# Two attention steps at a time in the prologue, and the second MLP's quotient held in PSUM

## The chip, the core and the metric

One core of one Trainium2 chip. The metric is the device time of one execution in microseconds (us). TensorE does matrix products, VectorE (DVE), ScalarE (ACT) and GpSimd (POOL) elementwise work, SyncE (SP) issues the DMAs. TensorE, VectorE and ScalarE reach PSUM, the accumulators' memory (eight banks of 128 x 512 floats here); all compute engines read SBUF.

## The reference

An attention layer followed by two MLPs. Attention: 2 batches, 8 heads, 768 positions, head size 64.

```python
scores = scale * q @ k.T
keep = (pos_k < n_global) | ((rel >= 0) & (rel < n_local))     # 8 and 96
scores = scores - slope[head] * dist                           # where keep, else -1e9
x = softmax(scores) @ v                                        # -> 1536 x 512
h = x @ w_in1                                                  # 512 -> 2048
x = (max(h, 0) + alpha * min(h, 0)) @ w_out1                   # 2048 -> 512
h = x @ w_in2
P = a0 + a1*h + a2*h**2 + a3*h**3
Q = 1 + |b0|*|h| + |b1|*h**2
out = (P / (Q + 1e-6)) @ w_out2
```

## The kernel before

**Tiling.** The 1536 tokens are three blocks of 512. A block has 4 tiles of 128 tokens and 4 pairs of heads, hence 16 attention steps (`STEPS`). A step reads its own tile of keys and the one before, 256 keys (128 in the first tile of the sequence, steps 0 to 3). Each MLP layer works on a block in 16 units m of 128 hidden features: hidden product h(m), gate g(m), split of g into a rounded part `g_hi` and a rest `g_lo`, output product y(m). Every product is made of three products of rounded parts (hi*hi, hi*lo, lo*hi), so h(m) and y(m) have 12 matmuls of 128 x 512 each.

**Stages.** The prologue does the attention of block 0 alone. Then layer 1 runs over three blocks, with the attention of the next block woven in between the matmuls of the first two, then layer 2 over three blocks. In layer 1 h runs two units ahead of y, in layer 2 three (`AHEAD`).

**Prologue.** `prologue_events` gives one order of events that TensorE, ScalarE and VectorE each follow, in program order. In turn s: transpose of the probabilities of step s-3 (`turn_prob`; TensorE L514, copied to SBUF by ScalarE L710), exponentials of s-1 (`exp`, ScalarE L702), scores of s (`score`, TensorE L500 and L502, with VectorE's shift L946), normalising of s-1 (`norm`, VectorE L954, behind the sum L987 and the inverse L991), output of s-3 (`attend`, TensorE L526, ScalarE L715, VectorE L961). Scores stand in four PSUM banks, transposes and outputs in two places each. ScalarE also makes the bias tables (L695), eight parts for steps 0 to 3 before the first exponential, and four pairs of a second table among steps 1 to 4.

**Loads.** SyncE issues all DMAs in its order: q and k of two steps (L377 to L380, once the scores up to two steps before are done), v (L390, L392, once an earlier step has attended), and pieces of 512 KB of the first layer's weights (L405), four of them at once at the start, the others when GpSimd has freed a stage. GpSimd rounds a piece (L1283) and forms the rest (L1247, L1250), one piece after the other. The last six pieces stand ahead of the q and k of block 1, which are issued in a loop.

**Gate of layer 2** for unit m: ScalarE makes h squared (L753), `q_abs` (L756), `denom` (L760), `numer` (L764) and `p_low` (L768) from the PSUM bank of h(m); GpSimd adds and multiplies them in SBUF (L1257, L1259, L1262); VectorE takes the reciprocal of `denom` (L1042), then forms `g_lo` of the unit before (L1054), then the quotient (L1048); ScalarE rounds the quotient to `g_hi` (L774). The banks of h are used by turns of four.

**Output product** (`output`, L606 and L608): y(m) waits for `g_lo` of m, which is the last part of g, then for each of four accumulator banks j does hi*hi, hi*lo, lo*hi. In the last unit TensorE signals after banks 0 and 1 (`y_half_done`) and at the end; ScalarE (L843) and VectorE (L1142) copy two banks each, and SyncE sends them out (L455).

Of the kernel before, what the change touches and what calls it, by code (L numbers as in the profile page):

```python
# [19 lines left out]
F32 = mybir.dt.float32  # L20
# [3 lines left out]
ALU = mybir.AluOpType  # L24
# [5 lines left out]
P = 128  # L30
# [5 lines left out]
BT = TOK // P  # L36
# [27 lines left out]
def build_program(nc, q, k, v, reach, w_in1, w_out1, alpha, w_in2, w_out2, ab, out):  # L64
    ctx = ExitStack()
    with ctx:
# [61 lines left out]
        negmax = sb("negmax", [P, 2, 2], F32)  # L128
        rowsum = sb("rowsum", [P, 2, 2, 2], F32)
# [20 lines left out]

        def in_block0(ab):
            return isinstance(ab, int)
# [114 lines left out]
        def prologue_events():  # L267


            for s in range(STEPS + 3):  # L270
                if s >= 3:
                    yield "turn_prob", s - 3
                if 1 <= s <= STEPS:
                    yield "exp", s - 1
                if s < STEPS:
                    yield "score", s
                if 1 <= s <= STEPS:
                    yield "norm", s - 1
                if s >= 3:
                    yield "attend", s - 3  # L280
# [75 lines left out]
        def _(sp):  # L356
# [10 lines left out]
            def load_qk(ab, i, batch, t):  # L367
                s = STEPS * ab + i
                slot, early = (i // PAIRS) % 2, in_block0(ab) and i < PAIRS
                two, loaded = slice(i % PAIRS, i % PAIRS + 2), (i % PAIRS) // 2  # L370
                tile = slice(t * P, (t + 1) * P) if isinstance(t, int) else bass.ds(t * P, P)
# [10 lines left out]
            def load_v(ab, i, batch, t):  # L382
                s = STEPS * ab + i
                slot, early = (i // PAIRS) % 2, in_block0(ab) and i < PAIRS
                loaded = (i % PAIRS) // 2
                tile = slice(t * P, (t + 1) * P) if isinstance(t, int) else bass.ds(t * P, P)
# [25 lines left out]
            load_piece(order1, 0, 1)  # L412
# [3 lines left out]
            for i in range(2, 4):  # L416
                load_piece(order1, 0, i)
            def due(i):

                return len(stage1) + (i - 2) * WHOLE // STEPS  # L420


            for i in range(PAIRS, STEPS, 2):
                load_qk(0, i, 0, i // PAIRS)
                for piece in range(due(i - 2), due(i)):
                    load_piece(order1, 0, piece)
                if i > PAIRS:
                    load_v(0, i - 2, 0, (i - 2) // PAIRS)
            load_v(0, STEPS - 2, 0, BT - 1)
            for piece in range(due(STEPS - 2), 2 * PIECES):  # L430
                load_piece(order1, 0, piece)
            with sp.Fori(0, BLOCKS - 1) as blk:
                def tile_at(i):

                    (b0, t0), (b1, t1) = (divmod(BT * r + i // PAIRS, TPB) for r in (1, 2))
                    return blk * (b1 - b0) + b0, blk * (t1 - t0) + t0

                load_qk(blk + 1, 0, *tile_at(0))
                for i in range(2, STEPS, 2):
                    load_qk(blk + 1, i, *tile_at(i))  # L440
                    load_v(blk + 1, i - 2, *tile_at(i - 2))
                load_v(blk + 1, STEPS - 2, *tile_at(STEPS - 2))
# [48 lines left out]
        def _(pe):  # L491
# [68 lines left out]
            def hidden(layer, blk, m, half, order, wait_w):  # L560
# [5 lines left out]
                if half == 0:  # L566
# [21 lines left out]
            def output(layer, blk, m, half, order, wait_w, after):  # L588

                c = MC * (blk + BLOCKS * layer) + m  # L590
                if half == 0 and layer == 1:
                    pe.wait_ge(g2_ready, MC * blk + (m + 1))
                elif half == 0:
                    pe.wait_ge(g_ready, c + 1)
                if half == 0:
                    if wait_w:
                        pe.wait_ge(w_ready, 2 * PIECES * layer + consumed_piece(order, m))
                for j in range(2 * half, 2 * half + 2):
                    if m == 0:
# [754 lines left out]
```

## Time and profile before

| | us |
|---|---|
| median of 3 runs (lowest, highest) | 672.76 (672.68, 672.94) |
| profiled execution, its own time | 673.6 |
| span in the profile | 671.9 |
| TensorE busy | 637.6 (95%) |
| VectorE busy | 500.8 (75%) |
| ScalarE, GpSimd busy | 321.0 (48%), 316.6 (47%) |
| mean granted TensorE clock | 0.988 of full |

Busy time of matmuls overlaps, since they are pipelined: a matmul of 128 x 512 is 0.39 us long and the next starts 0.227 us later. Places in the program are read from the timeline, whose times count from the start of the span. The profiled execution took 0.84 us more than the median.

### The profile page before, as it was taken

To read this page: it belongs to the slowest core of one execution; us is meant where nothing else is said; L and a number is where in the kernel's file an instruction comes from. 1 tells how busy PE (TensorE), PEld (TensorE's weight loads), DVE (VectorE), ACT (ScalarE), POOL (GpSimd) and SP (SyncE) were. 2 spreads that over 40 slices of the span, in tenths; PEclk is the share of its full clock that TensorE was granted. 3 is DMA by queue.
4 is the path that set the end of the run, shared out by engine and by line. 5 is a ranking of instruction groups with operands and counts; after the bars stand their busy time and mean duration, and the time that the engine had idled before them with its cause. 6 is when DMAs were issued, how large, how long until landed. Compare 5 with 4: busy or idle time off the path is not lost.

```text
span 671.9 us, 9562 instructions
## 1 busy us (share of the span) xinstructions
PE 637.6 (95%) x3048; PEld 506.4 (75%) x3048; DVE 500.8 (75%) x763; ACT 321.0 (48%) x664; POOL 316.6 (47%) x225
## 2 busy tenths in 40 slices
PE   3986999999999999999999998999999999999986
PEld 2665777777877777778888886888878887778864
DVE  6673766666376666645455569999989999899994
ACT  5671333333143323222111175777777777777772
POOL 5989200000000000001444486888878888788882
PEclk9997999999999999999999998999999999999998
DMA  6774121111000111010323210000010000100001
GB/s 202 200 232 126 32 52 28 28 45 40 0 27 27 46 36 28 9 48 16 102 95 114 98 32 0 1 1 0 1 63 0 0 0 0 62 1 0 1 0 65
DMA packets 38931, 31.26 MB, mean 47 GB/s; under 512 B 9008, under 2 KB 33264, under 8 KB 38896
## 3 DMA queue, kind: packets, MB, share of 16 engines
q1 hardware_dynamic: 38896, 30.83, 15.2%
q8 instruction: 18, 0.29, 0.2%
q14 instruction: 17, 0.14, 0.1%
HBM read 27.67 MB, written 3.15 MB: 46 GB/s over the span
## 4 chain that ended last, share of the span: by engine, by line
PE 76%; POOL 9%; ACT 5%; issue 3%; DMA 3%; SPq 2%; DVE 1%; POOLq 0%; ACTq 0%; DVEq 0%
PE ps_h L583 26%; PE ps_y L606 19%; PE ps_y L608 13%; PE ps_s L535 4%; POOL denom L1257 4%; POOL numer L1259 4%; PE ps_s L583 3%; PE ps_o L556 3%; PE ps_o L583 2%; DMA kT<-in_k 2%; PE ps_o L545 2%; ACT denom L760 2%; PE ps_y L502 2%; ACT h_sq L753 1%; SPq L377 1%
## 5 line engine op out<-in xcount | busy, mean ns | idle before, releaser
L1042 DVE RECIPROCAL denom<-denom 128x512 f32<-128x512 f32 x48 | 160.4, 3341 | 10.2 <-POOL denom L1257 10.2
L1250 POOL TENSOR_TENSOR win_lo<-stage,win_hi 128x1024 fp32r<-128x1024 f32 x8 | 19.2, 2402 | 265.4 <-DVE win_hi L1019 265.4
L583 PE MATMUL ps_h<-xy_hi,win_hi 128*128 (+1 forms) x288 | 119.2, 414 | 0.7 <-DVE xy_lo L961 0.7
L583 PE MATMUL ps_h<-xy_lo,win_hi 128*128 (+1 forms) x288 | 113.1, 393 | 0.0
L583 PE MATMUL ps_h<-xy_hi,win_lo 128*128 (+1 forms) x288 | 112.9, 392 | 0.0
L1257 POOL TENSOR_TENSOR denom<-denom,q_abs 128x512 f32<-128x512 f32 x48 | 79.0, 1646 | 39.5 <-ACT denom L760 39.5
L740 ACT ACTIVATE g_hi<-g 128x512 fp32r<-128x512 f32 x48 | 30.3, 631 | 138.3 <-PE ps_y L606 128.6
L608 PE MATMUL ps_y<-wout_hi,g_hi 128*128 128x512 f32 x192 | 77.7, 405 | 8.8 <-DVE g_lo L1054 8.8
L1036 DVE TENSOR_TENSOR g_lo<-g,g_hi 128x512 fp32r<-128x512 f32 x48 | 33.5, 697 | 65.9 <-ACT g_hi L740 65.9
L1259 POOL TENSOR_TENSOR numer<-numer,h_sq 128x512 f32<-128x512 f32 x48 | 80.3, 1672 | 3.7 <-ACT numer L764 3.7
L606 PE MATMUL ps_y<-g_hi,wout_hi 128*128 128x512 f32 x192 | 80.8, 421 | 0.0
L1048 DVE TENSOR_TENSOR numer<-numer,denom 128x512 f32<-128x512 f32 x48 | 76.5, 1593 | 0.1
L608 PE MATMUL ps_y<-wout_hi,g_lo 128*128 128x512 f32 x192 | 76.4, 398 | 0.0
L608 PE MATMUL ps_y<-wout_lo,g_hi 128*128 128x512 f32 x192 | 76.1, 397 | 0.0
L606 PE MATMUL ps_y<-g_lo,wout_hi 128*128 128x512 f32 x192 | 75.2, 392 | 0.0
L606 PE MATMUL ps_y<-g_hi,wout_lo 128*128 128x512 f32 x192 | 75.1, 391 | 0.0
L1262 POOL TENSOR_TENSOR numer<-numer,p_low 128x512 f32<-128x512 f32 x48 | 63.5, 1323 | 3.8
L583 PEld LDWEIGHTS ps_h<-xy_hi,win_hi 128*128 128x128 f32 x288 | 54.6, 190 | 14.1 <-issue 2.7
L583 PEld LDWEIGHTS ps_h<-xy_hi,win_lo 128*128 128x128 f32 x288 | 54.4, 189 | 11.7
L583 PEld LDWEIGHTS ps_h<-xy_lo,win_hi 128*128 128x128 f32 x288 | 54.5, 189 | 10.2
L1027 DVE TENSOR_SCALAR g<-ps_h,alpha_sb 128x512 f32<-128x512 f32 x48 | 36.0, 750 | 28.9 <-PE ps_h L583 28.9
L608 PEld LDWEIGHTS ps_y<-wout_hi,g_hi 128*128 128x128 f32 x192 | 36.6, 191 | 23.0 <-DVE g_lo L1054 16.1
(138 smaller groups left out, 1170.5 us busy)
## 6 DMA issues: line engine op xcount, KB each, us to landing
stage<-in_w_in SPq DMA_DIRECT2D x8, 512.0 KB, 3.4
stage<-in_w_out SPq DMA_DIRECT2D x8, 512.0 KB, 3.3
qT<-in_q SPq DMA_DIRECT2D x48, 64.0 KB, 2.4
kT<-in_k SPq DMA_DIRECT2D x24, 128.0 KB, 2.3
vv<-in_v SPq DMA_DIRECT2D x24, 128.0 KB, 2.2
out<-xy_raw SPq DMA_DIRECT2D x12, 256.0 KB, 2.2
xy_raw<-in_w_in SPq DMA_DIRECT2D x4, 512.0 KB, 5.7
xy_raw<-in_w_out SPq DMA_DIRECT2D x4, 512.0 KB, 5.6
```

Source lines behind the costliest of these rows:

```text
L535: mm = pe.matmul(ps_s[:, 2 * P * h:2 * P * (h + 1)], qT[:, pair, h, :], kT[:, pair].rearrange("d s t -> d (s t)"), start=True, stop=True)
L583: mm = pe.matmul(ps_h_at(layer, m), w[:, kc, cut], x[:, blk, kc, :], start=(kc == 0 and n == 0), stop=(kc == KC - 1 and n == 2))
L606: mm = pe.matmul(ps_y[:, j, :], w[:, m, cut], g[:, m % 2, :], **flags)
L608: mm = pe.matmul(ps_y[:, j, :], g[:, m % 2, cut], w[:, m, :], **flags)
L740: act.activation(g_hi[:, m % 2, :], g1[:, :], ACT.Copy).then_inc(g_hi_ready, 1)
L1027: dve.tensor_scalar(g1[:, :], ph, 0.0, alpha_sb[:, m:m + 1], ALU.min, ALU.mult).then_inc(neg_part, 1)
L1036: dve.tensor_tensor(g_lo[:, m % 2, :], g1[:, :], g_hi[:, m % 2, :].bitcast(F32), ALU.subtract).then_inc(g_ready, 1)
L1042: dve.reciprocal(denom[:, r, :], denom[:, r, :]).then_inc(inverse_ready, 1)
L1048: dve.tensor_tensor(numer[:, r, :], numer[:, r, :], denom[:, r, :], ALU.mult).then_inc(ratio_ready, 1)
L1257: pool.tensor_tensor(under, under, q_abs[:, :], ALU.add).then_inc(denom_ready, 1)
L1259: pool.tensor_tensor(top, top, h_sq[:, :], ALU.mult).then_inc(numer_high, 1)
L1262: pool.tensor_tensor(top, top, p_low[:, :], ALU.add).then_inc(numer_ready, 1)
```

## The change

Four things are edited.

1. The prologue's events come for two steps at a time: both transposes, both exponentials, both scores, both norms, both outputs. A step is transposed and attended in the turn of two after its norm. `negmax` and `rowsum` get four places instead of two. ScalarE makes four parts of the first bias table before the first exponential, the other four among the exponentials of steps 0 and 1, and the second table among those of steps 2 to 5. VectorE's preparation of the second distance table is cut in two (`later_keep`, `later_distances`).
2. SyncE's program has no loop: all three blocks of loads are written out, one weight piece at the start, then one piece per two steps in block 0 and two per two steps in block 1, behind the q, k and v of the turn.
3. An output product does its eight matmuls with `g_hi` first and waits only for `g_hi`; the four with `g_lo` come last, behind a wait for `g_lo`. `y_half_done` is signalled after the lo matmul of bank 1.
4. In layer 2 the reciprocal, the quotient and the source of `g_hi` and `g_lo` are in the PSUM bank of h(m), no longer in `denom` and `numer`. The reciprocal therefore waits for ScalarE's last read of that bank (`h_read`); ScalarE may write `denom` after the reciprocal and `numer` after the quotient of two units before; h(m+4) waits for `g_lo` of m.

```diff
-            for s in range(STEPS + 3):
-                if s >= 3:
-                    yield "turn_prob", s - 3
-                if 1 <= s <= STEPS:
-                    yield "exp", s - 1
...
+            for s in range(0, STEPS + 4, 2):
+                for i in (0, 1):
+                    if s >= 4:
+                        yield "turn_prob", s - 4 + i
+                for i in (0, 1):
+                    if 2 <= s <= STEPS:
+                        yield "exp", s - 2 + i
+                for i in (0, 1):
+                    if s < STEPS:
+                        yield "score", s + i
+                for i in (0, 1):
+                    if 2 <= s <= STEPS:
+                        yield "norm", s - 2 + i
+                for i in (0, 1):
+                    if s >= 4:
+                        yield "attend", s - 4 + i
...
+            piece = 1
+            for at_block in range(BLOCKS):
+                for i in range(0 if at_block else PAIRS, STEPS + 2, 2):
+                    if i < STEPS:
+                        load_qk(at_block, i, *divmod(BT * at_block + i // PAIRS, TPB))
+                    if i > (0 if at_block else PAIRS):
+                        load_v(at_block, i - 2, *divmod(BT * at_block + (i - 2) // PAIRS, TPB))
+                    if i < STEPS:
+                        for _ in range(2 if at_block else 1):
+                            if piece < 2 * PIECES:
+                                load_piece(order1, 0, piece)
+                                piece += 1
...
-                        pe.wait_ge(h_read, c2 - 3)
+                        pe.wait_ge(g2_ready, c2 - 3)
...
+                passes = [(j, w, g_hi) for j in range(KC) for w in (wout_hi, wout_lo)] + [(j, wout_hi, g_lo) for j in range(KC)]
+                for n in range(half * len(passes) // 2, (half + 1) * len(passes) // 2):
+                    j, w, g = passes[n]
+                    if m == 0 and n in (0, 2, 4, 6):
...
+                    if n == 2 * KC and layer == 1:
+                        pe.wait_ge(g2_ready, MC * blk + (m + 1))
...
+                    if after is None and m == MC - 1 and n == 2 * KC + 1:
+                        mm.then_inc(y_half_done, 1)
...
-                    act.wait_ge(ratio_ready, u - 1)
+                    act.wait_ge(inverse_ready, u - 1)
...
-                    act.wait_ge(g2_ready, u - 1)
+                    act.wait_ge(ratio_ready, u - 1)
...
-            for head in range(HEADS):
+            for head in range(4):
                 first_bias(head, slice(3 * P, 4 * P), D_FIRST)
...
-                if what == "exp" and 1 <= arg <= PAIRS:
+                if what == "exp" and arg < 2:
+                    for head in (2 * arg + 4, 2 * arg + 5):
+                        first_bias(head, slice(3 * P, 4 * P), D_FIRST)
+                elif what == "exp" and arg < 2 + PAIRS:
...
-                dve.reciprocal(denom[:, r, :], denom[:, r, :]).then_inc(inverse_ready, 1)
+                dve.wait_ge(h_read, MC * blk + (m + 1))
+                dve.reciprocal(ps_h_at(1, m), denom[:, r, :]).then_inc(inverse_ready, 1)
...
-                dve.tensor_tensor(numer[:, r, :], numer[:, r, :], denom[:, r, :], ALU.mult).then_inc(ratio_ready, 1)
+                dve.tensor_tensor(ps_h_at(1, m), numer[:, r, :], ps_h_at(1, m), ALU.mult).then_inc(ratio_ready, 1)
```

**TensorE in the full-width part of the prologue.** Before, one step after another (here the transposes of step 5, the scores of step 8, the outputs of step 5; then 6, 9, 6):

```order
L514 MATMUL ps_s<-ident,prob 128x128 [waits probT_ready,prob_ready]
L514 MATMUL ps_s<-ident,prob 128x128 x3
L502 MATMUL ps_y<-kT,qT 128x256 [waits prob_ready,qk_in0]
L502 MATMUL ps_y<-kT,qT 128x256
L526 MATMUL ps_o<-xy_raw,vv 64x128 [waits x_ready,v_in0,probT_ready]
L526 MATMUL ps_o<-xy_raw,vv 64x128 x3
L514 MATMUL ps_h<-ident,xy_raw 128x128 [waits probT_ready,prob_ready]
L514 MATMUL ps_h<-ident,xy_raw 128x128 x3
L502 MATMUL ps_y<-kT,qT 128x256 [waits prob_ready,qk_in0]
L502 MATMUL ps_y<-kT,qT 128x256
L526 MATMUL ps_h<-probT,vv 64x128 [waits x_ready,v_in1,probT_ready]
L526 MATMUL ps_h<-probT,vv 64x128 x3
```

Now (transposes of steps 4 and 5, scores of 8 and 9, outputs of 4 and 5):

```order
L500 MATMUL ps_h<-ident,prob 128x128 [waits probT_ready,prob_ready]
L500 MATMUL ps_h<-ident,prob 128x128 x3
L500 MATMUL ps_s<-ident,prob 128x128 [waits probT_ready,prob_ready]
L500 MATMUL ps_s<-ident,prob 128x128 x3
L488 MATMUL ps_y<-kT,qT 128x256 [waits prob_ready,qk_in0]
L488 MATMUL ps_y<-kT,qT 128x256
L488 MATMUL ps_y<-kT,qT 128x256 [waits prob_ready,qk_in0]
L488 MATMUL ps_y<-kT,qT 128x256
L512 MATMUL ps_h<-probT,vv 64x128 [waits x_ready,v_in0,probT_ready]
L512 MATMUL ps_h<-probT,vv 64x128 x3
L512 MATMUL ps_o<-xy_raw,vv 64x128 [waits x_ready,v_in0,probT_ready]
L512 MATMUL ps_o<-xy_raw,vv 64x128 x3
```

The groups of two steps stand together, and the transposes of a step come one turn of two after its norm.

**SyncE at the end of the prologue's loads.** Before, from the last v of block 0 to the first q of block 1, which is in the loop:

```order
L390 DMA vv<-in_v 128x256 [waits attended]
L392 DMA vv<-in_v 32x256
L405 DMA xy_raw_lo<-in_w_in 128x4x256 [waits w_ready]
L405 DMA xy_raw_lo<-in_w_out 128x2x512 [waits w_ready]
L405 DMA xy_raw<-in_w_in 128x4x256 [waits w_ready]
L405 DMA xy_raw<-in_w_out 128x2x512 [waits w_ready]
L405 DMA xy_raw_lo<-in_w_in 128x4x256 [waits w_ready]
L405 DMA xy_raw_lo<-in_w_out 128x2x512 [waits w_ready]
L432 UNCONDITIONAL_BRANCH
L432 ISA
L377 ISA [waits scored]
```

Now:

```order
L392 DMA vv<-in_v 128x256 [waits attended]
L394 DMA vv<-in_v 32x256
L379 DMA qT<-in_q 64x2x128 [waits scored]
L379 DMA qT<-in_q 64x2x128
L380 DMA kT<-in_k 128x2x128
L382 DMA kT<-in_k 128x2x32
L407 DMA xy_raw_lo<-in_w_out 128x2x512 [waits w_ready]
L407 DMA xy_raw<-in_w_in 128x4x256 [waits w_ready]
L379 DMA qT<-in_q 64x2x128 [waits scored]
```

Six pieces, each behind a wait for GpSimd, stood ahead of block 1's first q and k; now none of the last nine does.

**An output product of layer 2 on TensorE.** Before:

```order
L608 MATMUL ps_y<-wout_hi,g_hi 128x512 [waits g2_ready]
L608 MATMUL ps_y<-wout_hi,g_lo 128x512
L608 MATMUL ps_y<-wout_lo,g_hi 128x512
L608 MATMUL ps_y<-wout_hi,g_hi 128x512
L608 MATMUL ps_y<-wout_hi,g_lo 128x512
L608 MATMUL ps_y<-wout_lo,g_hi 128x512
```

The other six rows repeat these. Now:

```order
L599 MATMUL ps_y<-wout_hi,g_hi 128x512 [waits g2_hi_ready]
L599 MATMUL ps_y<-wout_lo,g_hi 128x512
L599 MATMUL ps_y<-wout_hi,g_hi 128x512
L599 MATMUL ps_y<-wout_lo,g_hi 128x512
L599 MATMUL ps_y<-wout_hi,g_hi 128x512
L599 MATMUL ps_y<-wout_lo,g_hi 128x512
L599 MATMUL ps_y<-wout_hi,g_hi 128x512
L599 MATMUL ps_y<-wout_lo,g_hi 128x512
L599 MATMUL ps_y<-wout_hi,g_lo 128x512 [waits g2_ready]
L599 MATMUL ps_y<-wout_hi,g_lo 128x512 x3
L569 MATMUL ps_h<-xy_hi,win_hi 128x512 [waits g2_ready]
```

The wait at the front is for `g_hi`; the one for `g_lo` stands behind eight of the twelve matmuls.

## Rows read from the trace of the kernel before

**Rows 1.** Timeline, prologue: start us, length us, engine, line, operation, count [idle before].

```profile
25.38 0.66 PE L514 MATMUL ps_h<-ident,prob 128*128 128x128 f32 x4
...
33.57 0.66 PE L514 MATMUL ps_h<-ident,prob 128*128 128x128 f32 x4
...
34.06 1.03 PE L502 MATMUL ps_y<-kT,qT 128*128 128x256 f32 x4
...
34.22 0.16 DVE L991 RECIPROCAL rden<-den 128x2 f32<-128x2 f32 x1
34.26 0.60 ACT L710 ACTIVATE probT<-ps_h 128x512 f32<-128x512 f32 x1 [0.29 <-PE ps_h L514]
34.48 0.69 DVE L954 TENSOR_TENSOR prob<-ps_y,rden 128x512 f32<-128x512 f32 x1
...
35.02 0.67 PE L526 MATMUL ps_h<-probT,vv 128*64 128x128 f32 x8
...
35.57 0.21 ACT L702 ACTIVATION_READ_ACCUMULATOR ps_y<-ps_y,negmax 128x1 f32 x1
...
46.76 0.66 PE L514 MATMUL ps_h<-ident,xy_raw 128*128 128x128 f32 x4
```

**Rows 2.** Timeline: first 256-key scores, and the second bias table on ScalarE.

```profile
17.74 2.08 PE L502 MATMUL ps_y<-kT,qT 128*128 128x256 f32 x4 [4.08 <-DMA kT<-in_k]
...
22.28 0.94 ACT L695 ACTIVATE bias<-dist 128x384 bf16<-128x384 bf16 x2
```

**Rows 3.** Timeline: end of the prologue and first attention step of the loop.

```profile
52.05 0.50 PE L583 MATMUL ps_h<-xy_hi,win_hi 128*128 128x512 f32 x1 [0.71 <-DVE xy_lo L961]
...
60.95 2.07 PE L535 MATMUL ps_s<-kT,qT 128*128 128x256 f32 x4 [4.49 <-DMA kT<-in_k]
...
62.46 0.99 PE L583 MATMUL ps_h<-xy_hi,win_hi 128*128 x1
```

**Rows 4.** Timeline of layer 2, third block: one unit on VectorE.

```profile
645.41 3.34 DVE L1042 RECIPROCAL denom<-denom 128x512 f32<-128x512 f32 x1
...
648.67 0.62 DVE L1054 TENSOR_TENSOR g_lo<-numer,g_hi 128x512 fp32r<-128x512 f32 x1
...
649.22 1.77 DVE L1048 TENSOR_TENSOR numer<-numer,denom 128x512 f32<-128x512 f32 x1
```

**Rows 5.** Timeline of the turn from layer 1 to layer 2.

```profile
396.36 1.73 DVE L1054 TENSOR_TENSOR g_lo<-numer,g_hi 128x512 fp32r<-128x512 f32 x1 [1.21 <-ACT g_hi L774]
...
397.62 1.62 POOL L1262 TENSOR_TENSOR numer<-numer,p_low 128x512 f32<-128x512 f32 x1
...
398.01 2.47 DVE L1066 TENSOR_TENSOR xy_lo<-ps_y,xy_hi 128x512 fp32r<-128x512 f32 x4
...
404.69 0.63 ACT L774 ACTIVATE g_hi<-numer 128x512 fp32r<-128x512 f32 x1 [3.38 <-DVE numer L1048]
...
407.84 1.20 DVE L1054 TENSOR_TENSOR g_lo<-numer,g_hi 128x512 fp32r<-128x512 f32 x1
...
410.28 2.19 DVE L1130 TENSOR_TENSOR wout_lo<-stage,wout_hi 128x1024 fp32r<-128x1024 f32 x1
```

**Rows 6.** Waits of TensorE, 63 us to the end: total us, times, longest us.

```profile
PE ps_y L608 <- DVE g_lo L1054: 8.8, 5, 3.1
```

**Rows 7.** Critical chain around the same turn: start us, us, what.

```profile
409.09 4.62 PE ps_y L608 x12
...
419.34 2.72 PE ps_s L583 x12
```

**Rows 8.** Timeline of TensorE, start of the second block of layer 2.

```profile
499.44 0.50 PE L608 MATMUL ps_y<-wout_hi,g_hi 128*128 128x512 f32 x1 [1.20 <-DVE g_lo L1054]
```

**Rows 9.** Timeline of the tail.

```profile
654.85 0.50 PE L608 MATMUL ps_y<-wout_hi,g_hi 128*128 128x512 f32 x1 [2.50 <-DVE g_lo L1054]
```

**Rows 10.** Timeline of the tail, VectorE evictions, then the output DMA issues.

```profile
666.13 0.69 DVE L1142 COPY xy_raw<-ps_y 128x512 f32<-128x512 f32 x1 [0.67 <-PE ps_y L608]
```

**Rows 11.** Timeline of the output DMA issues on the SyncE queue.

```profile
665.39 2.20 SPq L455 DMA_DIRECT2D out<-xy_raw  x4
```

More of the change, by code:

```diff
@@ L590, in output @@
                 c = MC * (blk + BLOCKS * layer) + m
[L591 to L594, printed above, removed]
                 if half == 0:
+                    if layer == 1:
+                        pe.wait_ge(g2_hi_ready, MC * blk + (m + 1))
+                    else:
+                        pe.wait_ge(g_hi_ready, c + 1)
                     if wait_w:
                         pe.wait_ge(w_ready, 2 * PIECES * layer + consumed_piece(order, m))
-                for j in range(2 * half, 2 * half + 2):
-                    if m == 0:
+                passes = [(j, w, g_hi) for j in range(KC) for w in (wout_hi, wout_lo)] + [(j, wout_hi, g_lo) for j in range(KC)]
@@ L601, in output @@
+                for n in range(half * len(passes) // 2, (half + 1) * len(passes) // 2):
+                    j, w, g = passes[n]
+                    if m == 0 and n in (0, 2, 4, 6):
                         pe.wait_ge(y_read, (blk + BLOCKS * layer) * KC + (j + 1))
[L602 to L608 removed]
+                    if n == 2 * KC and layer == 1:
+                        pe.wait_ge(g2_ready, MC * blk + (m + 1))
+                    elif n == 2 * KC:
+                        pe.wait_ge(g_ready, c + 1)
+                    flags = dict(start=(m == 0 and n < 2 * KC and n % 2 == 0), stop=(m == MC - 1 and n >= 2 * KC))
+                    cut = slice(j * P, (j + 1) * P)
+                    if layer == 0:
+                        mm = pe.matmul(ps_y[:, j, :], w[:, m, cut], g[:, m % 2, :], **flags)
+                    else:
+                        mm = pe.matmul(ps_y[:, j, :], g[:, m % 2, cut], w[:, m, :], **flags)
+                    if after is None and m == MC - 1 and n == 2 * KC + 1:
+                        mm.then_inc(y_half_done, 1)
@@ L609, in output @@
                 if half == 1:
                     mm.then_inc(y_done, 1)
-                elif after is None and m == MC - 1:
-                    mm.then_inc(y_half_done, 1)
             def run_block(layer, blk, attention, after, wait_w, wait_next):
@@ L1073, in _ @@
                     first_shift(arg, 0)
-                    if arg:
-                        denominator(0, arg - 1)
                     first_shift(arg, 1)
-                    if arg:
-                        inverse(0, arg - 1)
-                    else:
+                    if arg == 1:
+                        later_keep()
+                    if arg == 3:
                         later_distances()
-                elif what == "norm":
-                    if arg == STEPS - 1:
-                        denominator(0, arg)
-                        inverse(0, arg)
+                elif what == "norm" and arg % 2 == 0:
+                    denominator(0, arg)
+                    denominator(0, arg + 1)
+                    inverse(0, arg)
+                    inverse(0, arg + 1)
                     first_normalised(arg)
+                    first_normalised(arg + 1)
                 elif what == "attend":
```

70 lines of the change are left out of this document (17 added, 53 removed).

## Prediction

> **What bounds the kernel now.** I read the page first: TensorE is busy 95% of the span, so only what makes it wait, or run at its low clock, is worth anything. Then its waits, then the chain that ended last, then the timelines of the four places where these put the lost time. The reader is to see there:
>
> - In the prologue TensorE waits 4.08 us for k of step 4 [rows 2], which stands behind four weight pieces in the DMA queue, and at its end 4.49 us for k of block 1 [rows 3], which stands behind six pieces, each with a wait for GpSimd. Between them a step costs (46.76 - 25.38) / 10 = 2.14 us from the transposes of step 4 to those of step 14 [rows 1], close to TensorE's own work in a step: transposes 0.49 (33.57 to 34.06), scores 0.96 (to 35.02), outputs 0.67, together 2.12.
> - From 63 us on TensorE's waits are 8.8 us, five of them, all of y(m) for `g_lo` in layer 2 [rows 6]: 3.1 at the turn from layer 1, 1.20 at the second block [rows 8], 2.50 in the tail [rows 9], the other two 2.0 together.
> - A unit of layer 2 in the second and third block takes VectorE 645.41 to 648.67 for the reciprocal (3.26), 0.55 for `g_lo`, and, the quotient being 1.77 long, about 1.69 until the next one: 5.50 [rows 4]. TensorE needs 2 x 2.72 = 5.44 for h and y [rows 7]. So VectorE sets the pace there, by 0.06 us a unit.
>
> **The change part by part.** All sums are against the profiled execution, 673.6 us with a span of 671.9.
>
> *Quotient in PSUM.* It removes a second SBUF input from the quotient and from `g_lo`. The quotient is 1.77 long while GpSimd computes [rows 4]. The nearest rows with one PSUM and one SBUF input are the four `xy_lo`: 2.47 us together, 0.62 each, although a GpSimd operation ran through their first 1.2 us [rows 5]. I take 0.65 for both new forms; bounds are 0.62 and 1.77. A unit on VectorE becomes 3.26 + 0.65 + 0.65 = 4.56, well under 5.44. A reciprocal that writes PSUM is not in this trace; between no difference and 0.2 us more (that would still leave VectorE 0.7 us under TensorE) I take none. The added wait for `h_read` asks for ScalarE's last read of the bank, 2 x 0.77 or so behind `denom`, while GpSimd still needs 1.3 to 1.7 for its addition to `denom`: hidden. Behind the reciprocal on VectorE stand `g_lo` and the quotient, for which ScalarE and TensorE wait; the cover that pays if I am wrong is the three units that h runs ahead. The wait of h(m+4) for `g_lo` of m costs nothing, since y(m) has just been issued on it.
>
> The Trainium skill, "VectorE: DVE Perf Modes", section on the TRN2 errata, speaks against the move: a VectorE instruction pays a fixed 120 cycles from PSUM and 58 from SBUF. By it quotient and `g_lo` would be longer by 62 cycles of 0.96 GHz, an estimate of 0.06 us each, and a unit 4.7: no change in the sum.
>
> *Output product hi first.* y(m) can begin with `g_hi` and needs `g_lo` only 8 matmuls, 1.81 us, later.
>
> At the turn: `g_hi` of unit 1 is there at 404.69 + 0.63 = 405.32 [rows 5], y(1) began at 409.09 and took 4.62 us instead of 2.72, at the low clock [rows 7]. It can now follow h(4) at about 405.9. The first `g_lo`, 1.73 long [rows 5], falls to 0.65, which pulls all that VectorE does behind it 1.0 us forward, so `g_lo` of unit 1 ends near 409.0 - 1.0 - 0.6 = 407.4, in time. y(1) ends at 408.6, h(5) at 411.3. Late next is `g_lo` of unit 2: behind 407.4 VectorE has a quotient 0.65, a rounding of weights 0.7, `wout_lo` 2.19 [rows 5], a reciprocal 3.26 and itself 0.65: 414.9. y(2) ends 0.9 later, at 415.8, where it ended at 419.34 before [rows 7]. Gain 3.5.
>
> From there TensorE has 42 h and 45 y, 87 x 2.72 = 236.6 us. Before, from 419.34 to the last matmul's end, when VectorE's last eviction began at 666.13 [rows 10], less about 0.1, it took 246.7. The difference of 10.1 is the two waits at block starts and the slack 0.06 x 28 units, the two waits of the tail, and low clock after the 2.50 wait. All have their cover now but the last: behind the end of h(15), y(12) to y(14) take 8.16, and the chain of unit 15 is 3.35 to GpSimd's sum, 3.26, 0.65, 0.65 and 0.75 for `g_hi`: 8.65. So 0.5 stays, gain 9.6. Sum for layer 2: -13.1.
>
> *Tail.* `y_half_done` moves from 6 matmuls before the end to 2, that is 0.9 us later; the four output DMAs take SyncE 2.20 [rows 11], which started 0.7 before the end of y and will start 0.2 behind it. Cost +0.9.
>
> *Loads.* k of step 4 now follows one piece, not four: its scores start near 13.3 instead of 17.74 (-4.4). Block 1's k no longer waits: the 4.49 us go, and the low clock after them, scores 1.51 instead of 0.96 (60.95 to 62.46 [rows 3]) and some 1.3 us in the h behind: 6.3 us in all. Pieces come later, but none before it is needed: piece 8 is due at unit 6, 40 us into the loop, and I expect GpSimd done with it by 62 us.
>
> *Pairs.* Here the change costs. In a full-width turn of two, ScalarE does two copies and two steps of exponentials between the transposes of one turn and the norm of the same turn, and the next turn's transposes wait for that norm. From rows 1: transposes to the first copy 34.26 - 33.57 = 0.69; copy and exponentials of one step 34.26 to 35.78 = 1.52, twice 3.04; two sums and two inverses, 0.16 each and 0.26 from the second inverse to the norm, 0.55; the norm 0.69; together 5.0. TensorE's work in a turn is 4.1 to 4.2 and does not set the end. Before, norm and transposes lay a whole turn further apart, so this chain was covered. Five such turns from step 4 to step 14: 25.1 against 21.4, +3.7. The two turns before it carry the second bias table, 4 x 0.94 [rows 2], on the same ScalarE chain: 5.0 + 1.9 + shifts 0.2 = 7.1 for the second; from 13.3 I get the transposes of step 2 at 18.8 (at half speed, as the 2.08 of [rows 2] against 1.03) and those of step 4 at 25.9, against 25.38. So the DMA gain at the start is used up (+0.5 net), and 52.05 [rows 3] becomes 56.3. The 18 matmuls behind it take 4.4, then block 1's scores follow at once: 60.7, where before the loop began at 60.95 and lost 1.85 to the clock, as if at 62.8. Net for prologue and loads: -2.1. The unknown is the turn of two: bounds 4.1 (TensorE alone) and 5.9 (k of the turn after next is issued only after outputs, v and a piece: 3.7 of issue, then 2.4 to 4.0 to land), hence 56 or 65 for the loop's start.
>
> Sum: 673.6 - 13.1 + 0.9 - 2.1 = 659.3. The median of the runs lies 0.84 under the profiled execution, so 658.5.
>
> **Rivals.**
> - *Pairs as fast as TensorE.* If ScalarE's exponentials overlap its copies more than rows 1 show, a turn is 4.1 to 4.2: 5 x 0.9 less, 654.0. Against it: in rows 1 ScalarE works back to back from 34.26 to 35.78.
> - *Loads set the turn.* 5.9 a turn gives 5 x 0.9 more, 663.0. For it: 4.08 and 4.49 us of waits for k already [rows 2, 3]. Against: fewer pieces at once.
> - *The port is not freed.* If GpSimd still stretches the quotient to 1.77, VectorE stays at 5.5 a unit; the 1.7 of slack, and about 2 in the tail, come back: 662.2. Against it the `xy_lo` of [rows 5].
> - *The other side: the prologue stays at the low clock.* Each turn leaves TensorE idle for 0.9 of 5.0 us. Should the clock therefore not rise, a step is 0.98 + 1.92 + 1.2 = 4.1 and a turn 8.2; over six turns +19, giving 677.7. It decides from 2.4 us a turn on. Against it: at half speed the same work would fill the turn, and full-width scores went from 2.08 to 1.03 [rows 1, 2] once the work was dense.
>
> The Trainium skill, "TensorE: Matmul & The Clock Gate", section on the HAM clock gate, says the clock is set by how busy the array has been recently and halves after idleness. Trace and rule agree at the turn, where a wait of 3.1 us was followed by 4.62 for 12 matmuls [rows 6, 7]; for idle pieces of 0.9 us no run here shows it, and this rival is what the rule makes of them if they count.
>
> **How the numbers follow.** Forecast as summed 0.55 (its own range 656 to 661.5), fast pairs 0.14, loads 0.17, port 0.08, low clock 0.04, and 0.02 for a loss of another kind. Range 653.5 to 664: it takes in the first three rivals. This kernel's measurement tells 0.2% from no change, 1.3 us. Faster 0.95, within 0.01, slower 0.04.
>
> **What would show it.** Right: in layer 2 the quotient 0.65 to 0.7 long everywhere, y and h at 2.72 each in all three blocks, a TensorE wait of 1 to 2 us inside y(2) for `g_lo` and less than 1 in the tail; in the prologue turns of 5 us with TensorE idle before the transposes, waiting for the norm; no wait at the loop's start. Wrong: transposes every 4.1 us per two steps, or waits for k; a quotient still at 1.7; matmuls at 1.2 GHz in the middle of the prologue; waits for `w_ready` in the loop, because GpSimd starts later.

## The result

| | median us (lowest, highest) | ratio to the kernel before, 95% interval |
|---|---|---|
| kernel before | 672.83 (672.68, 672.94) | |
| changed kernel | 666.18 (665.79, 666.53) | 0.9901 [0.9884, 0.9918] |

Faster by 6.65 us; forecast were 14.3 and a range of 653.5 to 664.0. The direction was right, the size was not, and the time lies outside the range. The profiled execution took 666.53 us with a span of 664.8, beside 673.6 and 671.9 before: -7.1 in either.

### The profile page after: what moved, and what is told of

Its sections match the earlier page's. It is cut to its first block, busy times and chain, and to the rows that moved or that the text cites. A ratio compares the mean times of both kernels' runs of the same rounds, so it can differ in the third digit from the quotient of the medians.

```text
span 664.8 us, 9458 instructions
## 1 busy us (share of the span) xinstructions
PE 633.5 (95%) x3048; PEld 509.8 (77%) x3048; DVE 466.2 (70%) x763; ACT 311.6 (47%) x664; POOL 283.1 (43%) x225
## 4 chain that ended last, share of the span: by engine, by line
PE 85%; DVE 6%; ACT 3%; issue 3%; POOL 2%; DMA 0%; DVEq 0%; POOLq 0%; ACTq 0%
PE ps_h L569 28%; PE ps_y L597 19%; PE ps_y L599 18%; PE ps_s L569 5%; PE ps_o L569 5%; PE ps_s L521 4%; PE ps_o L542 3%; PE ps_o L531 2%; ACT ps_y L693 1%; PE ps_y L488 1%; PE ps_h L500 1%; POOL numer L1258 1%; PE ps_s L500 1%; ACT bias L686 1%; DVE ps_y L944 1%
## 5 line engine op out<-in xcount | busy, mean ns | idle before, releaser
L1041 DVE RECIPROCAL ps_h<-denom 128x512 f32<-128x512 f32 x24 | 80.6, 3360 | 17.4 <-POOL denom L1256 16.9
L1256 POOL TENSOR_TENSOR denom<-denom,q_abs 128x512 f32<-128x512 f32 x48 | 63.0, 1312 | 69.7 <-ACT denom L751 69.7
L599 PE MATMUL ps_y<-wout_hi,g_hi 128*128 128x512 f32 x192 | 74.8, 390 | 0.0
L599 PE MATMUL ps_y<-wout_lo,g_hi 128*128 128x512 f32 x192 | 74.7, 389 | 0.0
L1258 POOL TENSOR_TENSOR numer<-numer,h_sq 128x512 f32<-128x512 f32 x48 | 62.0, 1292 | 0.0
L599 PE MATMUL ps_y<-wout_hi,g_lo 128*128 128x512 f32 x192 | 51.7, 391 | 2.1 <-DVE g_lo L1053 2.1
L719 ACT ACTIVATE probT<-ps_o 128x512 f32<-128x512 f32 x32 | 19.0, 594 | 73.7 <-PE ps_o L531 73.7
L1041 DVE RECIPROCAL ps_s<-denom 128x512 f32<-128x512 f32 x12 | 40.3, 3360 | 16.9 <-POOL denom L1256 16.7
L597 PE MATMUL ps_y<-g_lo,wout_hi 128*128 128x512 f32 x192 | 51.8, 392 | 0.0
```

The source lines that it names most:

```text
L597: mm = pe.matmul(ps_y[:, j, :], w[:, m, cut], g[:, m % 2, :], **flags)
L599: mm = pe.matmul(ps_y[:, j, :], g[:, m % 2, cut], w[:, m, :], **flags)
L1041: dve.reciprocal(ps_h_at(1, m), denom[:, r, :]).then_inc(inverse_ready, 1)
L1256: pool.tensor_tensor(under, under, q_abs[:, :], ALU.add).then_inc(denom_ready, 1)
L1258: pool.tensor_tensor(top, top, h_sq[:, :], ALU.mult).then_inc(numer_high, 1)
```

## The profile after

TensorE's row of the page and the clock granted to it, in 40 slices of 16.6 us each:

```profile
PE   3788999999999999999999999899999999999996
...
PEclk8798999999999999999999999899999999999998
```

The second and the fourth slice of the clock are at 7 and 8, inside the prologue. TensorE's waits over the whole span (total us, times, longest us):

```profile
PE ps_h L500 <- DVE prob L952: 10.6, 4, 5.5
PE ps_y L486 <- DMA kT<-in_k: 5.4, 1, 5.4
PE ps_h L500 <- DVE xy_raw L952: 4.5, 4, 2.2
PE ps_y L599 <- DVE g_lo L1053: 2.1, 2, 1.9
PE ps_o L531 <- DVE prob L994: 1.6, 3, 0.7
PE ps_h L569 <- DVE xy_lo L959: 0.7, 1, 0.7
```

Of k only the first load is waited for; the waits of [rows 2, 3] are gone. The 8.8 us of [rows 6] are 2.1. In their place stand 15.1 us of transposes waiting for the norm, in eight turns. The prologue on TensorE, timeline (transposes and scores; some rows of each turn left out):

```profile
14.71 0.66 PE L500 MATMUL ps_h<-ident,prob 128*128 128x128 f32 x2 [5.51 <-DVE prob L952]
...
15.59 3.62 PE L488 MATMUL ps_y<-kT,qT 128*128 128x256 f32 x8
...
20.93 0.44 PE L500 MATMUL ps_h<-ident,xy_raw 128*128 128x128 f32 x2 [0.88 <-DVE xy_raw L952]
...
27.27 1.12 PE L500 MATMUL ps_h<-ident,prob 128*128 128x128 f32 x4 [3.26 <-DVE prob L952]
...
29.03 3.62 PE L488 MATMUL ps_y<-kT,qT 128*128 128x256 f32 x8
...
34.62 0.66 PE L500 MATMUL ps_h<-ident,xy_raw 128*128 128x128 f32 x4 [0.54 <-DVE xy_raw L952]
...
39.57 0.66 PE L500 MATMUL ps_h<-ident,prob 128*128 128x128 f32 x4 [0.89 <-DVE prob L952]
...
49.47 0.66 PE L500 MATMUL ps_h<-ident,prob 128*128 128x128 f32 x4 [0.89 <-DVE prob L952]
...
54.28 1.11 PE L500 MATMUL ps_h<-ident,xy_raw 128*128 128x128 f32 x4 [2.20 <-DVE xy_raw L952]
```

From step 6 to step 12 a turn is (49.47 - 34.62) / 3 = 4.95 us with 0.89 idle: the forecast of 5.0. Three places are not as forecast: the scores of step 4, at 15.59 and not 13.3, behind transposes that waited until 14.71; the turn from step 4 to 6, 7.35 us with scores at half speed; and the transposes of step 14, again slow. Behind them h(0)'s second half, at 52.05 before [rows 3], starts at 60.20 and not at 56.3. The clock granted from step 4's transposes on (columns: stretch, its length, busy us and count of TensorE, its weight loads, VectorE, ScalarE, GpSimd, then the mean granted clock as a share of 2.4 GHz, DMA share, GB/s):

```profile
27.20:34.60 7.40, 6.81 (x32) 5.38 (x32) 3.76 (x18) 3.57 (x12) 4.47 (x3) 0.58 0.26 79
34.60:54.20 19.60, 14.68 (x120) 11.14 (x120) 13.21 (x57) 13.83 (x48) 10.18 (x6) 0.99 0.58 171
54.20:57.20 3.00, 2.92 (x16) 2.30 (x16) 1.02 (x4) 1.19 (x2) 1.31 (x2) 0.50 1.07 343
```

Behind the 3.26 and the 2.20 us of idle TensorE is at or near its lower level of 1.2 GHz; between them, with 0.89 idle in each turn, at 2.4. What was late at 14.71, timeline of VectorE and GpSimd:

```profile
10.26 2.39 DVE L917 TENSOR_SCALAR xy_raw_lo<-xy_raw_lo,nn 128x32 f32<-128x32 f32 x1
10.27 2.34 POOL L1249 TENSOR_TENSOR win_lo<-xy_raw,win_hi 128x1024 fp32r<-128x1024 f32 x1
```

An operation on 32 columns, 0.24 us long before, ends with GpSimd's tensor_tensor that began beside it. The same operation and GpSimd's first piece in the kernel before, timeline:

```profile
8.32 0.24 DVE L919 TENSOR_SCALAR xy_raw_lo<-xy_raw_lo,nn 128x32 f32<-128x32 f32 x1
...
9.57 1.04 POOL L1283 CAST win_hi<-xy_raw 128x1024 fp32r<-128x1024 f32 x1 [6.76 <-DMA xy_raw<-in_w_in]
10.69 2.35 POOL L1250 TENSOR_TENSOR win_lo<-xy_raw,win_hi 128x1024 fp32r<-128x1024 f32 x1
```

GpSimd's two operations moved forward by 0.42 us, VectorE's moved back by 1.94: it now stands behind the shift of step 3 (`later_distances`), and stood behind that of step 0.

In layer 2 a unit of the third block on VectorE reads as follows (before: [rows 4]):

```profile
633.86 3.36 DVE L1041 RECIPROCAL ps_h<-denom 128x512 f32<-128x512 f32 x1 [0.90 <-POOL denom L1256]
637.13 0.67 DVE L1053 TENSOR_TENSOR g_lo<-ps_o,g_hi 128x512 fp32r<-128x512 f32 x1
637.72 0.68 DVE L1047 TENSOR_TENSOR ps_h<-numer,ps_h 128x512 f32<-128x512 f32 x1
```

The quotient fell from 1.77 to 0.68, and VectorE idles 0.90 us in each 5.44. The turn from layer 1, the chain that ended last (before: [rows 7]; at the end of layer 1 the kernel before is 3.0 us earlier, its h at 389.70 and not 392.69):

```profile
414.17 3.35 DVE ps_o L1041
417.52 0.59 DVE g_lo L1053
418.11 0.04 issue
418.16 1.34 PE ps_y L599 x4
419.49 4.19 PE ps_s L569 x12
423.69 2.73 PE ps_y L599 x12
```

y(2) ends at 419.5; the h behind it takes 4.19 instead of 2.72 us. The tail (before: [rows 10, 11]):

```profile
658.03 1.29 DVE L1141 COPY xy_raw<-ps_y 128x512 f32<-128x512 f32 x2 [1.88 <-PE ps_y L599]
658.65 2.05 SPq L441 DMA_DIRECT2D out<-xy_raw  x4
```

Both banks of VectorE are copied in one go, and SyncE starts behind TensorE's end: from the start of VectorE's last copy to the span's end it is 6.8 us, where it was 5.8. Part of that can be scatter between traces: with the old order it is 6.3 in e1, with the new one 7.2, 7.4 and 7.0 in e2, e3 and e9.

The 7.1 us of span are therefore: end of layer 1 3.0 later (a forecast of 2.1 earlier), layer 2 11.1 shorter (13.1), tail 1.0 longer (0.9).

## The experiments

Twelve kernels were measured in three groups, e1 to e4, e5 to e8 and e9 to e12, each beside the kernel before. That kernel had medians of 674.1 to 674.5 us there, over 1 us above its first ones, so kernels of different groups are compared by their ratio to it, and steps by their traces. "Single" stands for attention steps one at a time in the prologue, as before.

| | us | ratio, 95% interval |
|---|---|---|
| e1 before + PSUM quotient | 669.54 | 0.9927 [0.9901, 0.9953] |
| e2 before + g_hi first | 671.60 | 0.9955 [0.9939, 0.9971] |
| e3 both | 664.16 | 0.9842 [0.9810, 0.9874] |
| e4 both, new loads (all but the pairs) | 653.35 | 0.9676 [0.9647, 0.9704] |
| e5 changed kernel, GpSimd waits | 664.15 | 0.9841 [0.9819, 0.9862] |
| e6 e5 + bias table early | 660.76 | 0.9785 [0.9757, 0.9812] |
| e7 e4, GpSimd waits | 652.61 | 0.9669 [0.9649, 0.9688] |
| e8 e4, last weights later | 649.93 | 0.9632 [0.9613, 0.9651] |
| e9 e7 and e8 together | 649.55 | 0.9630 [0.9611, 0.9649] |
| e10 e9, pieces later | 650.94 | 0.9651 [0.9632, 0.9671] |
| e11 e9, banks 0 and 1 earlier | 650.15 | 0.9637 [0.9616, 0.9658] |
| e12 changed kernel again | 665.72 | 0.9874 [0.9849, 0.9898] |

**e1, e2, e3: the parts of layer 2.** e1 takes the hunks of the diff on `inverse2`, `ratio2`, `split2` and their waits, e2 the one on `output`, e3 both.

> The kernel before with only the quotient, reciprocal and source of g_hi and g_lo moved to PSUM; prologue, loads and output order as before. Theory A (VectorE's pace is what layer 2 loses, and the second SBUF input is what slows the quotient): the quotient falls from 1.77 to 0.65-0.70 us everywhere, the waits of y for g_lo shrink from 8.8 to about 4 (the turn from layer 1 stays), 672.8 - 8.5 = about 664.3 us. Rival B (the order of y is what matters, since it moves the moment at which g_lo is wanted): the quotient is shorter but y still waits, 670 or more.

> The kernel before with only the order of the output product changed (g_hi matmuls first, g_lo last, y_half_done before the last two matmuls). Theory A: VectorE still needs 5.5 us a unit against 5.44 of TensorE, so the 1.8 us of later demand are gained once, at the end, less 0.9 for the later y_half_done, and some low clock after long waits goes: about 670.5 to 671.5 us. Rival B: the order carries the gain, 666 or less.

> The kernel before with both edits of the MLP part (PSUM quotient, g_hi first), its prologue and its loads unchanged. Theory A (the shortfall of the prediction lies mostly in the prologue): layer 2 and tail give what the profile after shows there, -11.1 + 1.0 = -10.1: 662.7 us, that is faster than the changed kernel at 666.2, so the new prologue with its loads is a loss of 3.5. Rival B (the prologue part is worth the 2.1 that was forecast and layer 2 gives less than its traces show, for instance because the turn is different when it comes at another time): 668 us.

e1 gave half of what was expected, 4.6 us. The quotient is 0.68 long everywhere, but y still waits 7.9 us, at the same places as in [rows 6, 8]. TensorE at the second block of e1:

```profile
498.65 0.50 PE L608 MATMUL ps_y<-wout_hi,g_hi 128*128 128x512 f32 x1 [1.26 <-DVE g_lo L1055]
```

That is the 1.20 of [rows 8] with VectorE idle for 0.9 us a unit: the wait at a block's start is not VectorE's pace, but the chain behind one unit, and only a later demand covers it. In e2 the quotient is still 1.77 long, the waits at the block starts are 0.2 and 0.3, and those of the turn and the tail stay. Each alone leaves most waits, together they leave 2.1 us; 4.6 and 2.5 add up to 7.1, together it is 10.0 (against 674.13 in its group). In e3's trace the gain is 9.5 us of span. So layer 2 and the tail give what the trace after says, and prologue and loads together are a loss. The ratios, 0.984 for e3 and 0.990 and 0.987 for the changed kernel (e12), say so with intervals that touch; the traces say it clearly: the last h of layer 1 starts at 389.71 in e3, as in the kernel before, and at 392.69 and 392.28 in the two of the changed kernel.

**e4: without the pairs.** The hunks on `prologue_events`, `negmax`, `rowsum`, the bias parts and the distance tables are left out.

> As the run before, with the new order of loads too, so that only the pairs (two attention steps at a time) are missing from the changed kernel. Theory A: scores of step 4 start near 13.4 us, step 4 to 14 keep 2.14 us a step, block 1's k is there in time: the loop's first scores near 52 us where before lost until an effective 62.8; 662.7 - 10.7 = 652.0 us. Rival B (loads set the turn without pairs): q and k of two steps, 3.7 us of issue and 2.4 to 4.0 to land, come every 5.9 us and not every 4.3, TensorE waits for k again and again: 661 us. Rival C (the pairs cost nothing, and the shortfall lies elsewhere): 666 us.

Theory A: 653.35, expected 652.0. The new loads alone are worth 10.8 us (664.16 to 653.35; forecast 4.4 + 6.3 = 10.7). The pairs cost 0.9901 - 0.9676 = 0.0225, 15 us, by the ratios (13 us with the 0.9874 of e12), and 10.7 between the profiled spans, 664.8 and 654.1, of which e4's is that of its slowest execution. B is seen in small: two waits for k, 1.7 us together. The trace has the collision too, on larger operations:

```profile
8.91 1.30 DVE L907 TENSOR_TENSOR dist<-xy_raw_lo 128x256 bf16<-128x256 f32 x1
10.01 2.39 POOL L1237 TENSOR_TENSOR win_lo<-xy_raw,win_hi 128x1024 fp32r<-128x1024 f32 x1
10.13 2.42 DVE L908 TENSOR_TENSOR dist<-xy_raw_lo 128x128 bf16<-128x128 f32 x1
```

Before, these took 0.42 and 0.28 and were over at 9.54, when GpSimd's first piece began at 9.57. SyncE issues that piece at 5.3 in every trace, but it does not land at one time: with the old load order GpSimd begins it at 9.57, 9.66, 9.75 and 9.85 (before, e1, e3, e2), with the new one, where the landing sets GpSimd's start, at 8.89, 8.91, 9.15, 9.40 and 9.90 (e4, e12, changed kernel, e8, e7).

**e5, e7: the collision taken away.** One line, ahead of GpSimd's pieces, in the changed kernel (e5) and in e4 (e7):

```diff
+            pool.wait_ge(dist_ready, 3)
             for n in range(2 * PIECES):
```

> The changed kernel with one line more: GpSimd does not begin its weight pieces before VectorE has made both distance tables. Theory A (VectorE's small operation on the distances took 2.39 us instead of 0.24 only because a GpSimd tensor_tensor ran beside it): it takes 0.24 again, the first transposes start at 14.71 - 2.15 = 12.6 us, the scores of steps 4 and 5 behind them, everything up to the loop by 2 us earlier, 666.2 - 2.1 = 664 us or the same ratio to the kernel before less 0.003. Rival B (k of step 4, not the norm, would be late next, or the low clock takes it back): 666 us.

> The kernel with everything of the change but the pairs (653.35 us, span 654.1), with GpSimd's wait for the distance tables. Theory A: the two distance operations that took 1.30 and 2.42 us take 0.42 and 0.28, the first transposes start near 10.9 and not 13.91 us; k of step 4 is late next (issued at 7.7, with 2.4 to 4 us to land), so 2.0 to 3.0 us less: 651 us. Rival B (VectorE was not held, or k takes all of it back): no change.

VectorE and TensorE in e5:

```profile
10.45 0.23 DVE L917 TENSOR_SCALAR xy_raw_lo<-xy_raw_lo,nn 128x32 f32<-128x32 f32 x1
...
24.86 1.11 PE L500 MATMUL ps_h<-ident,prob 128*128 128x128 f32 x4 [3.26 <-DVE prob L952]
...
51.87 0.66 PE L500 MATMUL ps_h<-ident,xy_raw 128*128 128x128 f32 x4 [2.20 <-DVE xy_raw L952]
```

0.23 again; the transposes of steps 4 and 14 come 2.4 us earlier than in the changed kernel, the last h of layer 1 2.9 earlier (389.82), and the ratio is 0.006 under that of the changed kernel, 0.003 under e12's, with overlapping intervals there. Theory A. In e7 the first transposes start at 10.88, not 13.91, and the loop's first scores at 50.60, not 54.71, but the median gained 0.7 us only, where 2 to 3 were expected: e8 and e4 have the same prologue, and e8's profiled execution has its first transposes at 10.87. And in e7's own trace the new line held nothing: GpSimd waited for the piece itself, when VectorE's tables had been made 0.4 us before (9.52).

```profile
9.90 1.04 POOL L1271 CAST win_hi<-xy_raw 128x1024 fp32r<-128x1024 f32 x1 [7.10 <-DMA xy_raw<-in_w_in]
```

So without pairs the collision falls out one way or the other, with the landing of the piece, and e7's trace shows an execution that would have escaped it anyway; the line shows at work in e5. With pairs it was there in both profiled executions, which is what e12 was run for:

> The changed kernel itself once more, as a reference on the same chip. Theory A: VectorE's small operation on the distances takes 2.4 us again because GpSimd's first piece is ready at the same moment; ratio to the kernel before 0.989 to 0.991, first transposes at 14.7 us. Rival B (the collision falls out one way or the other from execution to execution, as it did between two of the kernels without pairs): it takes 0.24 here, transposes near 12.6, and the time is 2 us lower.

```profile
10.24 2.16 DVE L917 TENSOR_SCALAR xy_raw_lo<-xy_raw_lo,nn 128x32 f32<-128x32 f32 x1
```

The turn from step 4 to 6 took 6.26 us in this trace and 7.35 in the first, TensorE being back at full clock sooner. 0.9874 against 0.9901 is also how far this ratio moves between two groups; the intervals overlap.

**e6: the idle time before step 4's transposes.** Both distance tables are made behind step 1's shift, and four of the eight parts of the second bias table come where ScalarE idled:

```diff
-                elif what == "exp" and arg < 2 + PAIRS:
+                if what == "exp" and 1 <= arg < 4:
...
-                    for head in (2 * arg - 4, 2 * arg - 3):
+                    for head in (range(4), (4, 5), (6, 7))[arg - 1]:
```

> As the run before, and the second bias table is made earlier: VectorE makes both distance tables in one go behind step 1's shift, ScalarE four pairs of parts behind the exponentials of step 1, where it idled for 5.6 us, and two each behind those of steps 2 and 3. Theory A (the 3.26 us of idle TensorE before the transposes of step 4 came from the bias parts on ScalarE's chain, and the low clock behind it from that idle time): the idle time falls to 0.9 to 1.5 us, the following turn takes 5.0 us and not 7.35, so 1.9 + 2.4 us less than the run before, 660 us. Rival B (the low clock at 27 to 35 us comes from the pairs as such, since each turn idles): the turn stays over 7 us and only 1.9 us are gained.

```profile
22.71 0.66 PE L500 MATMUL ps_h<-ident,prob 128*128 128x128 f32 x4 [1.38 <-DVE prob L952]
...
27.95 0.66 PE L500 MATMUL ps_h<-ident,xy_raw 128*128 128x128 f32 x4 [0.89 <-DVE xy_raw L952]
...
47.61 0.91 PE L500 MATMUL ps_h<-ident,xy_raw 128*128 128x128 f32 x4 [2.20 <-DVE xy_raw L952]
```

Idle 1.38 instead of 3.26, and the turn behind it takes 5.24 instead of 7.34 us (e5: 24.86 to 32.20). Theory A: 2.15 us at step 4's transposes and 2.1 in the turn behind, 4.26 at step 14. The loop gains 3.1 of them (61.04 to 57.97), since behind the 2.20 us of idle the transposes are slow here and were not in e5. With the collision gone, and the low clock too but for the transposes of step 14, the pairs still cost 8.0 us of span against e7 (659.0 and 651.0; ratios 0.9785 and 0.9669).

**e8: the turn to layer 2.** In e4, the last weight piece is rounded and its rest formed in the first block's loop, which is written out, and no longer ahead of it:

```diff
-                elif what == "done":
-
-                    weights(MC - 1)
...
+                        if blk == 0 and arg == 5:
+                            weights(MC - 1)
+                        elif blk == 0 and arg == 8:
```

> The kernel with everything of the change but the pairs, and VectorE rounds the last weight piece of layer 2 behind the gates of units 5 and 8 of the first block, not ahead of unit 3 at the turn. Theory A (the rounding and the rest of that piece, 3.5 us with their gaps, are what makes g_lo of unit 2 late by 1.9 us, and the 1.5 us of low clock behind it come from that wait): the wait and the slow 12 matmuls of 4.19 us go, 3.4 us less, 650 us. Rival B (GpSimd's chain of units 2 and 3 is as late as VectorE's, so g_lo of unit 2 or 3 waits for GpSimd instead): 1 us or less. Rival C (the low clock has another cause than the wait): 2.2 us less, the 4.19 stays.

The chain that ended last in e8, across the turn:

```profile
404.18 2.72 PE ps_s L564 x12
406.90 2.72 PE ps_y L594 x12
409.62 2.72 PE ps_o L564 x12
```

Theory A: no wait, no slow product, and against e7 the last matmuls start 3.1 us earlier (640.55, 643.67).

**e9: both fixes.** e7's line and e8's edit.

> Everything of the change but the pairs, with GpSimd's wait for the distance tables and the last weight piece of layer 2 rounded later. Theory A (the two gains stand in different stages and add): 649.9 less what the collision of the distances costs in the executions that have it, 0.7 in the medians so far (653.35 against 652.61) and 3.1 between the two profiled executions: 649 us, with a narrower spread. Rival B (the collision was not in most executions anyway): 649.9.

649.55, the fastest kernel here, 3.7% under the kernel before; not to be told from e8, whose profiled execution escaped the collision; that most of the others did too is likely (648.8 to 650.6 us, where e4 has 651.2 to 656.0) and not shown.

**e10: fewer issues ahead of k.**

```diff
-                        for _ in range(2 if at_block else 1):
+                        for _ in range(2 if at_block else int(i not in (8, 10))):
```

> As the run before, and no weight piece is issued behind the loads of steps 8 and 10, so SyncE has two issues of 0.47 us less ahead of the k of steps 10 and 12. Theory A (SyncE's issue of nine DMAs a turn, 3.95 of 4.28 us, is what makes k of steps 8 to 11 late by 0.9 to 1.3 us): the wait for k shrinks to under 0.4, 0.9 us less. Rival B (two more pieces then fall into the loop, where GpSimd's work stretches VectorE's operations ahead of the transposes): the waits for prob in the loop grow by as much, no change or 1 us more.

Rival B, by a different row than it named. The waits for k, 0.9 together, are 0.35, and the loop's first scores come 0.87 earlier (51.37 to 50.50); then, VectorE and TensorE:

```profile
50.29 2.53 DVE L1022 TENSOR_TENSOR g_lo<-g,g_hi 128x512 fp32r<-128x512 f32 x1 [0.77 <-ACT g_hi L726]
...
57.45 1.13 PE L516 MATMUL ps_s<-kT,qT 128*128 128x256 f32 x4 [1.81 <-DVE prob L962]
```

`g_lo` takes 2.53 and not 0.69 us, held by a piece of GpSimd (49.90 to 52.27), the next one 1.64, and the scores of step 1 wait 1.81 us for VectorE. The edit did more than move pieces: GpSimd forms the rest of the first eight pieces in one operation of 1024 columns each, and of the later ones in parts of 256. In e9 the piece at this place is a later one, in four parts (50.06 to 53.34), and the same `g_lo`, at 51.16, takes 0.88.

**e11: the tail.**

```diff
+                last = after is None and m == MC - 1
+                if last:
+                    passes = passes[:6] + passes[8:10] + passes[6:8] + passes[10:]
```

> As the first run of this call, but the last output product finishes banks 0 and 1 four matmuls before its end and not two (banks 0 to 2 with g_hi, g_lo of banks 0 and 1, bank 3, g_lo of banks 2 and 3), so that half of the result can leave earlier. Theory A (the 0.9 to 1.0 us of the tail come from y_half_done): the time from TensorE's end to the span's end falls from 6.8 to 6.2-6.4, while the wait for g_lo grows by 0.45, so 0 to 0.3 us less in all. Rival B (the span's end is set by the last two DMAs' landing alone): the wait grows and nothing is gained, 0.4 us more.

SyncE starts its output 0.34 us earlier (641.61, e9 641.95), VectorE's last copy starts 0.57 later (641.89, e9 641.32), spans are 648.4 and 648.3, the ratios overlap: no change. From that copy to the end it is 6.5 us for 7.0, so the order of the last product does set a part of the tail, but this way of getting it back costs as much.

## Why the prediction was wrong

By its own steps, against the profiled executions. It missed by 7.2 us (666.5, forecast 659.3). The step that failed is the net for prologue and loads, put at -2.1 and measured at +3.0. Two terms of it were at nothing: the stretching of VectorE's small distance operation by GpSimd (0.24 us, measured 2.39), and the low clock in the turn from step 4 to 6 (put at 5.0 us, measured 7.35).

1. *Quotient in PSUM*: right. 0.68 and 0.67 us for 0.65 (`g_lo` was 0.62 from SBUF [rows 4], so the 0.06 that the prediction set beside its sum is about there), VectorE needs 5.44 - 0.90 = 4.54 us a unit for 4.56. The rival of the port not freed is out.
2. *The turn from layer 1*: y(2) ended 2.9 us earlier for 3.5 (419.49 against 419.34 + 3.0), with a wait of 1.9 us inside it as foreseen. What was not priced is what this wait does to the clock, though the prediction names the same pair in the kernel before (3.1 us of wait, then 4.62 for a product): the h behind took 4.19 us, +1.5. e8 removed wait and slow product together.
3. *Steady state, boundaries and tail's stall*: gain 9.7 for 9.6, if the 1.5 is left with point 2 (658.03 - 419.49 = 238.5 to VectorE's last copy; before 666.13 - 419.34 = 246.8). But the reason given for the two waits at block starts was wrong in part: e1 shows that VectorE's pace is not their cause, g_hi first is what removes them.
4. *`y_half_done`*: +1.0 for +0.9, as near as traces of one order agree among themselves (5.8 and 6.3, 6.8 to 7.4).
5. *Loads*: right in size, 10.8 for 10.7, where nothing else takes the gain (e4). Loads never set the turn; that rival is out.
6. *Pairs, the turn of two*: 4.95 for 5.0, idle 0.89 for 0.9. The arithmetic of that chain held. Up to the loop's first scores the pairs cost 7.4 us in e6 against e7 (57.97, 50.60), where the forecast implied 60.7 - (62.8 - 10.7) = 8.6; but that one has 1.9 us of bias parts in it, which e6 moved away, and e6 has slow transposes at step 14, so the two agree only roughly.
7. *What it missed in the prologue*, 3.9 us (60.20 for 56.3). (a) +2.1: the distance operation now stands beside GpSimd's first piece, and e5 shows what that costs. Two edits brought them together: the pairs moved the operation back, from 8.32 to 10.26, and the load order can bring the piece forward, here from 9.57 to 9.15. The prediction speaks of neither. The first would have been enough, as far as the rows tell: e5's distance operations run from 10.45 to 11.67, and GpSimd's tensor_tensor at its old place, 10.69 to 13.04, would have met them. No run has the pairs with the old loads. (b) +2.4: the low clock behind the idle time before step 4's transposes. It follows from the prediction's own chain: the turn that ends with these transposes was put at 7.1 us with the bias parts in it, and TensorE's work in a turn is at most 4.2, hence 3 us idle. The rival of the low clock was asked of the turns of 0.9 us idle, where it never came, and priced for six of them alike, not for this one. e6 shows it. (c) +1.0: the same behind step 14's transposes, 5.92 us from there to 60.20 where e5 without it takes 4.91. Stretches shorter than forecast gave 1.6 back, the turn from step 2 to 4 above all, 6.34 for 7.1.
8. *Layer 1 behind it*, 1.2 us more: pieces that GpSimd works on in the loop stretch VectorE there. The transposes wait 1.6 us (0.7 in e3, whose loop has the old loads), behind rows as this one, 0.62 long where GpSimd is idle (at 89.32):

```profile
83.77 1.68 DVE L994 TENSOR_SCALAR prob<-prob,rden 128x256 f32<-128x256 f32 x2
```

"Pieces come later, but none before it is needed" was true and not the point. e10 shows the mechanism, not this size; about 0.3 us of the 1.2 stay unexplained.

Together: 3.9 + 1.2, 1.5 + 0.6 of point 2, and 0.1 of the tail less 0.1 of point 3, 7.2. The range failed because its upper end was the loads' rival, and no case held the collision or the low clock for one turn alone.

The Trainium skill, "SBUF — State Buffer", section "SBUF: two separate sides", says that GpSimd's operations and VectorE's with two SBUF inputs or in a two-port mode exclude each other for a whole instruction, the one that starts first holding the pair. The rows at 10.26 and 10.13 agree, 2.39 and 2.42 us against GpSimd's 2.34 and 2.39, though at 10.26 the two starts are 0.01 us apart and do not tell which was first; by this rule the collision could have been forecast from the new places of the two. For the clock, "TensorE: Matmul & The Clock Gate", section "What's actually happening", says that the same kernel can come out differently from run to run. The two traces of the changed kernel agree: behind the same 3.26 us of idle the turn from step 4 to 6 took 7.35 us in one, with a granted clock of 0.58, and 6.26 in the other (e12), with 0.76.

Not settled: whether the old loads with the pairs would have hidden the pairs' cost or kept the collision (not run), and how often the collision falls in executions that were not profiled.

## What to carry to other kernels

Price an idle piece of TensorE by what runs behind it too: here 3.26 us of idle cost 2.1 more at half clock, 0.89 cost nothing. When an edit moves an operation of VectorE back or a load forward, look at what VectorE and GpSimd will now do side by side, as much as at whom the load serves. Pairing steps lengthens the chain from one step's product to its use, and gains nothing where the steps already come at TensorE's own pace, as here at 2.14 us for 2.12.

## What the runs showed of the hardware

- A VectorE operation of 0.24 us took 2.39 beside a GpSimd tensor_tensor, 0.28 took 2.42, a `g_lo` of 0.69 took 2.53: the small one pays the length of the other, not a share of it.
- In the kernels without pairs, whether it happens can turn on half a microsecond of a DMA's landing: with the same prologue GpSimd's first piece began at 8.89 in e4 and at 9.40 in e8, the first transposes at 13.91 and 10.87.
- The same 2.20 us of idle were followed by a granted clock of 0.50 and 0.54 at once in the changed kernel (54.28 to 57.24) and e6 (47.61 to 50.40), of 0.88 and then 0.50 in e12 (from 54.29), and of 1.00 in e5 (51.87 to 53.80).
